# Moving the weighing products, the row sums, two softmaxes and the q/k loads inside the slots of a fused attention and MLP kernel

## The reference

```python
q_d, k_d, v_d = (mean over groups of 4 rows)        # 144 rows
out_d   = softmax(q_d k_d^T / 8) v_d                # pooled attention
out_up  = repeat each row of out_d 4 times
mask    = |i - j| < 4
out_loc = softmax(where(mask, q k^T / 8, -1e9)) v   # band of 7 keys for each query
x       = out_up + out_loc                          # heads side by side: (2304, 512)
x = (h * sigmoid(h)) @ w_out,  h = x @ w_in         # first MLP
x = (s * relu(h)^2 + b) @ w2_out,  h = x @ w2_in    # second MLP
```

## Time and profile before

| what | us |
|---|---|
| median of three runs | 980.44 |
| the three runs | 978.83, 980.44, 986.79 |
| the profiled execution, its own time | 979.32 |
| span of its profile (first to last instruction) | 977.5 |
| busy PE, POOL, DVE, ACT | 939.1, 459.5, 429.2, 375.0 |
| mean granted clock of TensorE | 0.988 |

### The profile page before, as it was taken

The page is one execution under the profiler, slowest core; times in us unless marked ns, Lnnn a source line. Parts: engine busy times, 40 slices in busy tenths (PEclk is TensorE's granted clock), DMA queues, the critical chain, the costliest instruction groups (busy, mean ns, idle before and its releaser), DMA issues.

```text
span 977.5 us, 15807 instructions
## 1 busy us (share of the span) xinstructions
PE 939.1 (96%) x6071; PEld 868.0 (89%) x6071; DVE 429.2 (44%) x909; ACT 375.0 (38%) x999; POOL 459.5 (47%) x444
## 2 busy tenths in 40 slices
PE   8999999599799999899999999999999999999998
PEld 8899999599799999899999988888888888888897
DVE  5577435626636546356464654224222322322232
ACT  5566443333343433434424553224223222322332
POOL 6767467658758668577474223222222222222222
PEclk9899999889999999999999999999999999999999
DMA  6655343242151343332203542002001100100010
GB/s 178 174 150 172 91 121 95 64 102 69 42 142 46 83 107 77 87 94 55 76 1 97 176 129 79 1 1 87 1 1 43 43 0 0 64 0 0 2 43 21
DMA packets 87170, 68.75 MB, mean 70 GB/s; under 512 B 38720, under 2 KB 73024, under 8 KB 87104
## 3 DMA queue, kind: packets, MB, share of 16 engines
q1 hardware_dynamic: 87104, 67.86, 25.2%
HBM read 52.76 MB, written 15.08 MB: 69 GB/s over the span
## 4 chain that ended last, share of the span: by engine, by line
PE 80%; DVE 5%; POOL 5%; issue 5%; ACT 3%; DMA 1%; SPq 0%; POOLq 0%; ACTq 0%; DVEq 0%
PE pH L796 20%; PE pY L811 20%; PE pH L739 15%; PE pY L744 14%; PE pS L587 3%; PE pO L633 2%; POOL x_hl L315 2%; POOL g_hl L315 1%; PE pS L590 1%; DVE w_in_hl L315 1%; DVE o_last L1271 1%; PE pO L639 1%; POOL weighted L1494 1%; DVE w_out_hl L315 1%; PE pO L671 1%
## 5 line engine op out<-in xcount | busy, mean ns | idle before, releaser
L315 POOL TENSOR_TENSOR g_hl<-act,g_hl 128x288 fp32r<-128x288 f32 (+2 forms) x208 | 199.8, 962 | 450.1 <-ACT g_hl L835 449.7
L744 PE MATMUL pY<-g_hl,w_out_hl 128*128 128x288 f32 x1536 | 238.1, 299 | 6.6 <-POOL g_hl L315 6.6
L739 PE MATMUL pH<-x_hl,w_in_hl 128*128 128x288 f32 x1518 | 233.8, 302 | 4.3 <-POOL x_hl L315 2.9
L744 PEld LDWEIGHTS pY<-g_hl,w_out_hl 128*128 128x128 f32 x1536 | 213.6, 189 | 7.8 <-POOL g_hl L315 7.8
L739 PEld LDWEIGHTS pH<-x_hl,w_in_hl 128*128 128x128 f32 x1518 | 214.1, 192 | 5.1 <-issue 4.3
L796 PE MATMUL pH<-x_hl,w_in_hl 128*128 128x512 f32 (+1 forms) x960 | 208.4, 368 | 0.0
L811 PE MATMUL pY<-w_out_hl,g_hl 128*128 128x512 f32 x864 | 207.8, 390 | 0.0
L796 PEld LDWEIGHTS pH<-x_hl,w_in_hl 128*128 128x128 f32 x960 | 169.0, 188 | 31.0
L811 PEld LDWEIGHTS pY<-w_out_hl,g_hl 128*128 128x128 f32 x864 | 161.2, 188 | 33.1 <-POOL g_hl L315 0.3
L835 ACT ACTIVATE g_hl<-act 128x288 fp32r<-128x288 f32 (+2 forms) x208 | 104.0, 500 | 194.5 <-DVE act L1383 103.7
L1381 DVE TENSOR_TENSOR act<-act 128x512 f32<-128x512 f32 (+1 forms) x80 | 55.5, 694 | 270.6 <-ACT act L1069 270.6
(11 more groups left out here) (139 smaller groups left out, 777.9 us busy)
## 6 DMA issues: line engine op xcount, KB each, us to landing
qk_f<-qk SPq DMA_DIRECT2D x32, 292.0 KB, 3.5
vd_f<-vp SPq DMA_DIRECT2D x64, 144.0 KB
stage_in<-w_in SPq DMA_DIRECT2D x32, 256.0 KB, 2.8
stage_out<-w_out SPq DMA_DIRECT2D x32, 256.0 KB, 3.0
v_loc<-vp SPq DMA_DIRECT2D x24, 240.0 KB, 4.6
score_bands<-act SPq DMA_DIRECT2D x48, 114.8 KB, 2.4
qk_f<-qk SPq DMA_DIRECT2D x64, 72.0 KB, 2.7
x_scratch<-y_sb SPq DMA_DIRECT2D x8, 576.0 KB, 3.8
```

Of the source, the lines that this page charges most:

```text
L315: eng.tensor_tensor(lo, full, hi.bitcast(F32), ALU.subtract).then_inc(signal, 1)
L739: last = pe.matmul(pH[:, f % 2, 0:T1], w_in[:, wp, c, f * P:(f + 1) * P], x1[:, par, mp, c, :], start=c + n == 0, stop=c == C - 1 and n == 2)
L744: last = pe.matmul(pY[:, c, 0:T1], w_out[:, wp, f, c * P:(c + 1) * P], g_hl[:, f % RING, mp, 0:T1], start=f + n == 0, stop=f == NF - 1 and ...
```

## The change

The tables tell for each slot in which of two places a product and in which of three places a sum stands. A slot's first products stand ahead of its first `g_low`, the second ones ahead of its other `g_low`, behind the unit's q, k and v sums. A slot's sums stand at its start, between the unit's `maxima` and `normalise`, or at its end. In tile 1 and tile 2 `row_shift` stands right behind the slot's first gate, `row_exps` behind its first `g_high`, and `row_normalise` in the same slot, behind the `maxima`. The q and k of unit k+2 are loaded in slot k in every slot with one unit, also across the tile's end, and in tile 2 the third turn stands at (7, 12). POOL takes the v sums of a pair's second unit in the next slot, behind that slot's q and k sums.

```diff
-WEIGH = {2: (0, 1), 3: (2, 3), 4: (4, 5), 5: (6, 7), 6: (8,)}
-WEIGH_IN = {1: {5: (0, 1, 2), 6: (3, 4, 5), 7: (6, 7, 8)}, 2: {3: (0, 1), 4: (2, 3), 5: (4, 5), 6: (6, 7, 8)}}
-SUM = {2: (0,), 3: (1, 2), 4: (3, 4), 5: (5, 6), 6: (7, 8)}
-SUM_IN = {1: {5: (0, 1, 2), 6: (3, 4, 5), 7: (6, 7, 8)}, 2: {3: (0,), 4: (1, 2), 5: (3, 4), 6: (5, 6, 7, 8)}}
-QK_AHEAD = {(1, 9): 0, (2, 9): 0, (1, 12): 2}
+WEIGH = {2: ((0,), (1,)), 3: ((2,), (3,)), 4: ((4,), (5,)), 5: ((6,), (7,)), 6: ((8,), ())}
+WEIGH_IN = {1: {4: ((), (0,)), 5: ((1, 2), (3,)), 6: ((4, 5), (6,)), 7: ((7, 8), ())},
+            2: {2: ((), (0,)), 3: ((1,), (2,)), 4: ((3,), (4,)), 5: ((5,), (6,)), 6: ((7, 8), ())}}
+SUM = {2: ((), (0,), ()), 3: ((1,), (2,), ()), 4: ((3,), (4,), ()), 5: ((5,), (6,), ()), 6: ((7,), (8,), ())}
+SUM_IN = {1: {5: ((0,), (1, 2), ()), 6: ((3,), (4, 5), ()), 7: ((6,), (7, 8), ())},
+          2: {3: ((0,), (1,), ()), 4: ((2,), (3,), ()), 5: ((4,), (5,), ()), 6: ((6,), (7,), (8,))}}
+QK_AHEAD = 2
-TURNS_IN = {1: {(6, 36): 0, (7, 2): 1, (7, 47): 2}, 2: {(5, 36): 0, (6, 36): 1, (7, 2): 2}}
+TURNS_IN = {1: {(6, 36): 0, (7, 2): 1, (7, 47): 2}, 2: {(5, 36): 0, (6, 36): 1, (7, 12): 2}}
...
 SP
-                                if w := unit(h, k + QK_AHEAD.get((t, k), 1)):
+                                if w := unit(h, k + QK_AHEAD):
                                     load_qk(w)
...
 ACT
                     g_high(L[0], t, f, 2, T1)
+                    if u == softmax_in(t) != SOFTMAX:
+                        row_exps(t, h)
...
-                    if u == softmax_in(t):
+                    if u == softmax_in(t) == SOFTMAX:
                         row_exps(t, h)
...
 DVE
-                    if u == softmax_in(t) + 1:
+                    if u - 1 == softmax == SOFTMAX:
                         row_normalise(t, h)
-                        sums = (None, *sums)
-                    for i in sums[:1]:
-                        if i is not None:
-                            sum_row(t, i)
+                    for i in sums[0]:
+                        sum_row(t, i)
...
                     gate1(t, UPS[u][0])
+                    if u == softmax != SOFTMAX:
+                        row_shift(t, h)
...
                     if not two and (w := unit(h, now[0])):
                         maxima(w)
+                    if u == softmax != SOFTMAX:
+                        row_normalise(t, h)
+                    for i in sums[1]:
+                        sum_row(t, i)
                     if w := unit(h, now[0]):
                         normalise(w)
...
-                    for i in sums[1:]:
+                    for i in sums[2]:
                         sum_row(t, i)
...
 POOL
                     if two:
                         qk_sums(unit(h, now[1]))
-                    for i in weigh_in(t, u)[:2]:
+                    if u and len(units(t, u - 1)) == 2:
+                        v_sums(unit(h, units(t, u - 1)[1]))
+                    for i in first:
                         weigh(t, i)
...
-                    for i in weigh_in(t, u)[2:]:
+                    for i in second:
                         weigh(t, i)
                     for f in UPS[u][1:]:
                         g_low(L[0], t, f, T1)
-                    if two:
-                        v_sums(unit(h, now[1]))
```

More of the change, by code:

```diff
@@ L341, in unit @@
             half, par, batch = h
-            if u >= H:
+            while u >= H:
                 half, par, batch, u = half + 1, 1 - par, batch + par, u - H
-                if isinstance(half, int) and half == HALVES:
-                    return None
+            if half >= HALVES:
+                return None
             return half * H + u, half, par, batch, u
@@ L355, in weigh_in @@
         def weigh_in(t, u):
-            return WEIGH_IN.get(t, WEIGH).get(u, ())
+            return WEIGH_IN.get(t, WEIGH).get(u, ((), ()))
         def sum_in(t, u):
-            return SUM_IN.get(t, SUM).get(u, ())
+            return SUM_IN.get(t, SUM).get(u, ((), (), ()))
         def softmax_in(t):
@@ L1288, in slot_rows @@
                     finish = u == H - 1 and not late(t, u)
+                    softmax = softmax_in(t)
                     if u == 1:
                         gate1(t, CARRIED)
-                    if u == softmax_in(t) + 1:
+                    if u - 1 == softmax == SOFTMAX:
                         row_normalise(t, h)
-                        sums = (None, *sums)
-                    for i in sums[:1]:
-                        if i is not None:
-                            sum_row(t, i)
+                    for i in sums[0]:
+                        sum_row(t, i)
                     if finish:
@@ L1306, in slot_rows @@
                         maxima(w)
+                    if u == softmax != SOFTMAX:
+                        row_normalise(t, h)
+                    for i in sums[1]:
+                        sum_row(t, i)
                     if w := unit(h, now[0]):
                         normalise(w)
-                    if u == softmax_in(t):
+                    if u == softmax == SOFTMAX:
                         row_shift(t, h)
@@ L1504, in slot_rows @@
                     two = len(now) == 2
+                    finish = u == H - 1 and not late(t, u)
+                    first, second = weigh_in(t, u)
                     if u == 1:
@@ L1508, in slot_rows @@
                         qk_sums(unit(h, now[1]))
-                    for i in weigh_in(t, u)[:2]:
+                    if u and len(units(t, u - 1)) == 2:
+                        v_sums(unit(h, units(t, u - 1)[1]))
+                    for i in first:
                         weigh(t, i)
-                    finish = u == H - 1 and not late(t, u)
                     if finish and (w := unit(h, now[0])):
```

## The result

The changed kernel takes 948.93 us (median of four runs, 947.60 to 949.76) where the kernel before takes 982.35 in the same set (978.83 to 986.79): ratio 0.966, 95% interval 0.961 to 0.970. The forecast was 952.0, range 944 to 963. The profiled execution took 947.6 with a span of 945.8, so 31.7 of span are gone.

What follows compares the result with a forecast made beforehand. TensorE bounds the kernel, so gains come only from its waits and the lower clock behind them: 13.0 + 7.6 + 7.8 = 28.4 off the profiled 979.3 gives 950.9, plus 1.1 for the median of runs 952.0, range 944 to 963.

Steps and rivals of the forecast that it cites:

- Tile 1, 7.8: Tile 1: turn waits 2.1, 3.4 and 2.0 go, a new 1.2 comes at down 15, 1.5 of lower clock goes.
- Tile 2, 7.6: Tile 2: 1.5 from the score wait, 4.65 from the third turn, 1.5 from the lower clock behind it.
- Tiles 3 to 6, 13.0: Tiles 3 to 6: 6.3 from turn waits, 5.1 from remainder waits, 1.6 from tile 5's lower clock.
- 4 x 1.6 = 6.3 gone: Third turns of tiles 3 to 6: sum 8 comes some 2 us earlier, so each turn's 1.6 wait goes.
- 5.1 gone: Starts of tiles 3, 4 and 5: earlier q and k loads remove TensorE's waits for the remainder g_low.
- The place of the products: Tiles 3 to 6: product 8 becomes the first thing in POOL's slot 6; no separate gain was listed.
- the cover of 5 us: Tiles 3 to 6: POOL's second remainder is ready about 5 us before TensorE asks, so mid-slot places cost 0.
- The rule against it: DVE operations with two SBUF inputs block beside POOL: down 15 of tile 1 up to 1.3 later, forecast 953.3.
- Rows late in tiles 1 and 2: Rival, chance 0.18: POOL over-full in tiles 1 and 2, half of 7.8 + 7.6 lost, 959.7.
- The load's wait stays: Rival, chance 0.05: SP, held by the bands, issues the load no sooner; 5.1 + 1.6 are kept, 958.7.
- The dips come anyway: Rival, chance 0.07: the lower-clock stretches remain though waits go; 1.5 + 1.5 + 1.6 are kept, 956.6.
- More goes: Rival, chance 0.12: tile 1's new 1.2 doesn't come, and 3.0 of lower clock at tile 2's start goes, 947.8.

Runs made afterwards that it cites:

- second profile of the changed kernel: The changed kernel run once more, unaltered, as the measure for a later set: 946.46 us, ratio 0.970 to the kernel before.
- e1_loads: The kernel before with only the earlier q and k loads (unit k+2 in slot k, also across a tile's end): 971.73 us, ratio 0.992.
- e3_late_tiles_alone: The kernel before with, in tiles 3 to 6 only, second products behind the unit's sums and second sums between maxima and normalise: 977.36 us, ratio 0.996.
- e11_loads_and_sums: The kernel before with the earlier loads and, in tiles 3 to 6, second sums between maxima and normalise, products unmoved: 965.47 us, ratio 0.984.
- e12_v_sums_behind: The changed kernel with the previous pair's v sums behind the q and k sums in the row-softmax slot of tiles 1 and 2: 947.7 us, one execution.
- the fillers: The changed kernel with 20 throwaway large matmuls while TensorE waits for x at tile 2's start: 944.59 us, ratio 0.968 to the kernel before.
- e2_all_but_loads: The changed kernel with the q and k loads of the kernel before: 964.39 us, ratio 0.984 to the kernel before.

## Why the prediction was right, and where a step was not

The time (948.9 for 952.0) and its sum came from the right stretches: 29.1 for 28.4. Of the 3.3 us between the profiled execution (947.6) and the 950.9 worked out for one, 2.6 lie in the start and in tile 7, which the change doesn't touch. By the prediction's steps:

- *Tile 1, 7.8*: measured 7.7. Gate 13, which came at 172.8, now starts at 169.3, and its g_high at 169.8; the first turn waits for nothing, the second 0.5, the third for nothing. The new wait at down 15 is 0.9 (1.2 forecast), and the clock behind the second turn is full. The 2.9 at tile 2 and the lower clock behind it stayed.
- *Tile 2, 7.6*: measured 6.9. The turn left 0.34 (0.4 forecast); the score wait went; the attend behind it waited 0.95 here and 0.33 in the second profile of the changed kernel, where 0.2 was taken.
- *Tiles 3 to 6, 13.0*: measured 14.4 (12.7 and 1.8). Most of the 1.4 between them is that a wait costs more than the idle that the profile prints: tile 6 loses one wait of 1.59 and is 1.77 shorter, and in `e1_loads` tiles 3 and 4 lose 1.69 and 1.12 and are 1.94 and 1.38 shorter. That is 0.2 more each time, and there are seven such waits.
- *The step that failed* is the split of that sum, "4 x 1.6 = 6.3 gone" by the sums and "5.1 gone" by the loads, each on its own. The total holds only because both edits are made. In tiles 3 to 5 the loads alone give 7.4, and both 12.7. The sums alone give 1.7 for each turn less the 1.0 that goes back into the next load's wait, and with the clock on top their tiles came out anywhere from 5.2 shorter to 2.7 longer in the profiles; over the whole kernel the runs of `e3_late_tiles_alone` are 4 us shorter, not 6.3, with 1.8 of it in tile 6. The 6.3 holds for the sums only where no load stands behind them: in tile 6, and with the loads moved (7.0 from `e1_loads` to `e11_loads_and_sums`). I had priced each wait by its own row, and had not asked of the first what SP's fixed list (band, windows, load) does once the turn is earlier.
- *The place of the products* in tiles 3 to 6 was carried at 0 and is 0; *the cover of 5 us* for the middle places held against a sum more in each (1.6 us in all), and for POOL the limit is not the remainder but the sum that waits for its product.
- *The rule against it* held, and more than was allowed for: not up to 1.3 once, but 2.1 on one operation and 0.8 on another (L1252: 1.00) in tile 1, and 2.1 in tile 2. Product 0 of tile 1 started at 157.3, which with the 1.1 that this execution was ahead is 1.2 later than worked out. Little of that is the standing still, since POOL's queue was nearly full up to there anyway: without the 2.1, in `e12_v_sums_behind`, product 0 is 0.3 sooner and the wait at down 15 is the same.
- *The rivals.* Rows late in tiles 1 and 2: not so. The load's wait stays: not so. The dips come anyway: not so; the three low stretches behind removed waits (the second turn of tile 1, the third of tile 2, the load of tile 5) are gone, as the rule of the Trainium skill, page "TensorE: Matmul & The Clock Gate", Part 1, would have it, and the fillers show the same from the other side. *More goes* came in neither of its parts, though the 948.9 is nearer to its 947.8 than to 952.0: by the profile that comes from the start and tile 7, not from its mechanism.

## What to carry to other kernels

Two waits in one loop that stand behind one another on the critical engine are not two gains: taking one away can hand part of its time to the other, so price each edit with the other in and out, or test both alone. An engine that issues in a fixed order (here SP: band, windows, load) deserves its own question: what does its next transfer hang on once the wait ahead is gone? And where an unavoidable wait of TensorE is followed by slow matmuls, throwaway matmuls in a free accumulator are cheap to try.

## What the runs showed of the hardware

- A VectorE operation with two SBUF inputs stood still beside GpSimd work for as long as that ran from one instruction to the next without a gap: 2.43 us for one of 0.29, over parts of three GpSimd instructions; and 1.43 for an x_add of 0.46. The sums, with one input, ran at 1.74 to 1.81 in the changed kernel beside products at 1.69 throughout. The Trainium skill, page "SBUF — State Buffer", section "SBUF: two separate sides", has the lock held for an instruction; here the waiting operation got in only at a gap between GpSimd's instructions, some 0.1 us before one that reads what the last one wrote.
- A tensor_scalar on 18 columns from SBUF took 0.82 us in `e12_v_sums_behind` while GpSimd was in its pair sum, and 0.18 in the changed kernel, though it has one input.
- The clock fell to 1.2 GHz behind waits of TensorE of 1.5 (tile 3 of `e3_late_tiles_alone`), 2.1 (first turn of tile 1 in `e1_loads`), 2.3 and 2.7 to 5.0 us. It stayed full behind others as long: 1.6 at the third turns, 2.1 at the first turn of tile 1 before, 2.7 in tile 4 of `e2_all_but_loads`. So the length of the wait alone does not decide it, and the prediction's "those of 2.0 had none" is no rule.
